# Other token pieces, sixteen places for whole weights and four stages for their splits, in an attention and two-MLP kernel

## What is computed

```python
kth = np.partition(scores, -32, axis=-1)[..., -32:-31]
scores = np.where(scores >= kth, scores, -1e9)
attn = np.exp(scores - np.max(scores, axis=-1, keepdims=True))
attn = attn / (np.sum(attn, axis=-1, keepdims=True) + 1e-09)
x = np.matmul(attn, v)                          # 2304 x 512 after the transpose
gate = 1 / (1 + np.exp(-(x @ w_gate)))          # 512 x 1536
y = (gate * (x @ w_val)) @ w_out                # 1536 x 512
r = np.maximum(y @ w_in, 0)                     # 512 x 2048
out = (r * r) @ w_out2                          # 2048 x 512
```

## Time and profile before

| | before |
|---|---|
| median of the runs shown | 1252.26 us |
| the profiled execution, own time | 1252.19 us |
| its span, first to last instruction | 1250.4 us |
| mean granted TensorE clock | 0.978 |
| PE matmul busy | 1169.2 us, 94% |
| DVE busy | 848.4 us, 68% |
| ACT busy | 740.7 us, 59% |
| POOL busy | 626.3 us, 50% |
| DMA | 270.13 MB, mean 216 GB/s |

### The profile page before, as it was taken

One profiled execution on the slowest core, in us unless ns is written; L12 is line 12 of the kernel. 1 busy time (PEld: TensorE's weight loads), 2 busy tenths in 40 slices (PEclk: granted clock), 3 DMA queues, 4 the chain that ended last, 5 costly groups with the idle time before them and its releaser, 6 DMA issues.

```text
span 1250.4 us, 21797 instructions
## 1 busy us (share of the span) xinstructions
PE 1169.2 (94%) x7520; PEld 991.9 (79%) x7520; DVE 848.4 (68%) x1756; ACT 740.7 (59%) x1758; POOL 626.3 (50%) x539
## 2 busy tenths in 40 slices
PE   3469989869999999999999999999999999999999
PEld 2248877769999898888888777777778788888999
DVE  7988988737779977788997667688864445610121
ACT  5777778557768756666776666467654443531221
POOL 4875668646648845553664445356543333530220
PEclk9769999989999999999999999999999999999999
DMA  7874667686665785655456555454555545556997
GB/s 262 313 266 143 230 209 225 204 298 225 224 228 199 246 309 192 198 199 170 160 191 230 200 168 191 168 185 153 175 193 194 178 160 181 176 189 212 365 369 263
DMA packets 89245, 270.13 MB, mean 216 GB/s; under 512 B 9904, under 2 KB 15024, under 8 KB 89136
## 3 DMA queue, kind: packets, MB, share of 16 engines
q1 hardware_dynamic: 89136, 268.74, 62.7%
HBM read 228.33 MB, written 40.37 MB: 215 GB/s over the span
## 4 chain that ended last, share of the span: by engine, by line
PE 80%; ACT 6%; POOL 4%; DMA 4%; DVE 4%; issue 2%; SPq 1%; ACTq 0%; DVEq 0%; POOLq 0%
PE ps L497 21%; PE ps L499 19%; PE ps L498 19%; PE ps L438 6%; PE ps L402 5%; PE ps L418 5%; PE ps L483 3%; DMA w_split<-ring 2%; POOL below L728 2%; DVE work L663 2%; DVE top L661 1%; POOL ring L723 1%; ACT scores L529 1%; DMA ring<-w_in 1%; ACT probs L548 1%
## 5 line engine op out<-in xcount | busy, mean ns | idle before, releaser
L728 POOL TENSOR_TENSOR below<-scores,below 128x576 f32<-128x576 f32 x144 | 205.2, 1425 | 297.9 <-ACT below L541 285.5
L661 DVE MAX8 top<-work 128x8 f32<-128x576 f32 x432 | 312.9, 752 | 5.0
L497 PE MATMUL ps<-xy_hi,ring 128*128 128x512 f32 (+3 forms) x800 | 292.1, 365 | 0.3 <-ACT act_buf L597 0.3
L499 PE MATMUL ps<-xy_hi,ring 128*128 128x512 f32 (+3 forms) x800 | 283.2, 354 | 0.0
L498 PE MATMUL ps<-xy_lo,ring 128*128 128x512 f32 (+3 forms) x800 | 283.2, 354 | 0.0
L663 DVE MATCH_REPLACE8 work<-top,work 128x576 f32<-128x576 f32 x288 | 213.8, 742 | 0.0
L497 PE MATMUL ps<-g_hi,ring 128*128 128x512 f32 (+3 forms) x560 | 203.0, 363 | 0.0
L499 PE MATMUL ps<-g_hi,ring 128*128 128x512 f32 (+3 forms) x560 | 197.8, 353 | 0.0
L498 PE MATMUL ps<-g_lo,ring 128*128 128x512 f32 (+3 forms) x560 | 197.6, 353 | 0.0
L497 PEld LDWEIGHTS ps<-xy_hi,ring 128*128 128x128 f32 x800 | 151.4, 189 | 24.8 <-issue 9.7
L687 DVE SCALAR_TENSOR_TENSOR full_buf<-act_buf,ps 128x512 f32<-128x512 f32 (+3 forms) x60 | 35.5, 591 | 193.1 <-PE ps L499 176.7
(11 more groups left out here) (56 smaller groups left out, 1749.9 us busy)
## 6 DMA issues: line engine op xcount, KB each, us to landing
ring<-w_split SPq DMA_DIRECT2D x318, 512.0 KB, 3.7
w_split<-ring SPq DMA_DIRECT2D x68, 512.0 KB, 4.2
ring<-w_in SPq DMA_DIRECT2D x113, 256.0 KB, 3.4
vt<-v_in SPq DMA_DIRECT2D x16, 480.0 KB, 5.3
heads_in<-qk_in SPq DMA_DIRECT2D x16, 336.0 KB, 4.8
vt<-v_in SPq DMA_DIRECT2D x16, 320.0 KB, 4.1
heads_in<-qk_in SPq DMA_DIRECT2D x16, 240.0 KB, 3.8
heads_in<-qk_in SPq DMA_DIRECT2D x8, 368.0 KB, 5.6
```

What stands on the lines that cost most here:

```text
L497: nc.tensor.matmul(dst, w_hi, hi[:, k, 0:WIDTH[c]], start=first, stop=False)
L499: mm = nc.tensor.matmul(dst, w_lo, hi[:, k, 0:WIDTH[c]], start=False, stop=final)
L661: nc.vector.max(out=best, in_=sc if step == 0 else wk).then_inc(sel_step[t % 2], 1)
L728: nc.gpsimd.tensor_tensor(out=below[:, t % 2, :], in0=scores[:, t % PLACES, :], in1=below[:, t % 2, :], op=ALU.subtract).then_inc(mask_don ...
```

## The change

The pieces become 128, 256, 384, 512, 512 and 512 tokens (2, 4, 6, 8, 8, 8 blocks of 64). NW = 1 names the number of pieces computed whole in float32 (it stays the first alone; x1 and the pieces of code for more of them are not used). Jobs before piece 1 (NWHOLE = 91 of them) now have 16 places of their own, of 2 KB per partition, in the same memory as the ring; their parts go to one of four stages of 4 KB, in memory of g_lo, which piece 0 does not use. The ring of 8 double places takes over from piece 1 on; job k >= 91 waits for the two whole places that its place covers. SP stores a stage three blocks after its block (STORE_LAG), ACT waits for the store of four splits before. POOL no longer waits for the block's matmuls, and waits once, in piece 1, for the last four stages' stores. probs_h has two places, and its memset is twice as long. The splits ahead of piece 0 begin in slot 0 and not in slot 2; at the start SP issues sixteen whole weights, eight before the second v and eight after it. JOBS, its number of splits (68) and of whole loads (113) stay as they are. With the pieces, MLP_AT goes from 16, 41, 69, 101, 133, 149 to 12, 29, 53, 85, 117, 149, and the groups from 32 to 36 (still 64 full and 16 half units).

```diff
-CHUNK_BLOCKS = (3, 6, 7, 8, 8, 4)
+CHUNK_BLOCKS = (2, 4, 6, 8, 8, 8)
+NW = 1
...
-RING = 8
+RING, WPLACES, STAGES = 8, 16, 4
 AHEAD = 5
+STORE_LAG = 3
+CLASSES = NW + 2
...
+NWHOLE = NPRE + NW * NB
...
+STAGED = [k for k in SPLITS if k < NWHOLE]
+STAGE_OF = {k: r for r, k in enumerate(STAGED)}
...
+RING0 = (NWHOLE + 1) % WPLACES // 2
+def ring_place(k):
+    return (k - NWHOLE + RING0) % RING
...
+def jobs_ahead(k):
+    if k < NWHOLE:
+        return [k - WPLACES] if k >= WPLACES else []
+    if k >= NWHOLE + RING:
+        return [k - RING]
+    return [i for i in range(NWHOLE - WPLACES, NWHOLE) if i % WPLACES // 2 == ring_place(k)]
+LOAD_AT = {}
+for _k in range(len(JOBS)):
+    if jobs_ahead(_k) and max(jobs_ahead(_k)) >= NPRE:
+        LOAD_AT.setdefault(max(jobs_ahead(_k)) + 1, []).append(_k)
+FIRST_LOADS = [k for k in range(NWHOLE) if not jobs_ahead(k)]
...
-    SPLIT_AT.setdefault(2 + _k // 2, []).append(_k)
+    SPLIT_AT.setdefault(min(2, MLP_AT[0] - (NPRE + 1) // 2) + _k // 2, []).append(_k)
...
-        probs_h = sb("probs_h", [P, SEQ + B64])
+        probs_h = sb("probs_h", [P, 2, SEQ + B64])
...
+        with nc.sbuf_tensor("stage", [P, STAGES, 2, KT * P], F32R) as stage, \
...
-        with nc.sbuf_tensor("ring0", [P, RING, 2, KT * P], F32) as ring0:
+        with nc.sbuf_tensor("wring", [P, WPLACES, KT * P], F32) as wring:
...
             def load_weights(k):
...
+                for ahead in jobs_ahead(k):
+                    if ahead >= NPRE:
+                        sp.wait_ge(blk_done, ahead - NPRE + 1)
+                    if JOBS[ahead][2] and ahead < NWHOLE:
+                        sp.wait_ge(w_lo_done, SPLIT_OF[ahead] + 1)
+                    elif JOBS[ahead][2]:
+                        wait_stored(sp, ahead)
...
-                    load_weights(k - 1 + RING)
-                    if k + AHEAD in SPLIT_OF and JOBS[k + AHEAD][0] == 1:
+                    for job in LOAD_AT.get(k, []):
+                        load_weights(job)
+                    if k + AHEAD in SPLIT_OF and JOBS[k + AHEAD][0] == NW:
                         store_parts(k + AHEAD)
-                    if c == 0 and k in SPLIT_OF:
-                        store_parts(k)
+                    if k - STORE_LAG in STAGE_OF and k - STORE_LAG >= NPRE:
+                        store_parts(k - STORE_LAG)
...
-            for k in range(RING):
+            for k in FIRST_LOADS[:RING]:
                 load_weights(k)
             load_v(1)
+            for k in FIRST_LOADS[RING:]:
+                load_weights(k)
...
             def split_weights(k):
-                act.wait_ge(ring_loaded[k % RING], 16 * (k // RING + 1))
-                nc.scalar.activation(place(k)[:, 0, :], whole(k), ACT.Copy).then_inc(w_hi_done, 1)
+                wait_loaded(act, k)
+                if k < NWHOLE and STAGE_OF[k] >= STAGES:
+                    wait_stored(act, STAGED[STAGE_OF[k] - STAGES])
+                nc.scalar.activation(both_parts(k)[:, 0, :], whole(k), ACT.Copy).then_inc(w_hi_done, 1)
...
                 pool.wait_ge(w_hi_done, SPLIT_OF[k] + 1)
-                if JOBS[k][0] == 0:
-                    pool.wait_ge(blk_done, k - NPRE + 1)
```

More of the change, by code:

```diff
@@ L171 @@
     HEADS_AT.setdefault(max(FIRST_TILE[_g - 1] - 3, 0), []).append(_g)
-for _c in range(1, NC):
+for _c in range(NW, NC):
     for _p in range(PAIRS):
@@ L242, in probs_of, with both_parts @@
             u, part = TILES[t]
-            return probs_h[:, 0:SEQ] if part == 2 else probs[:, RANK[u] % 2, part, :]
-        def place(k):
-            return ring[:, k % RING, :, :]
+            return probs_h[:, RANK[u] % 2, 0:SEQ] if part == 2 else probs[:, RANK[u] % 2, part, :]
         def whole(k):
-            return ring0[:, k % RING, 1, :]
+            return wring[:, k % WPLACES if k < NWHOLE else 2 * ring_place(k) + 1, :]
+        def both_parts(k):
+            return stage[:, STAGE_OF[k] % STAGES, :, :] if k < NWHOLE else ring[:, ring_place(k), :, :]
         const_step = sem("const_step")
@@ L256, in attention_mlps @@
         out_stored = [sem("out_stored0"), sem("out_stored1")]
+        whole_loaded = [sem(f"whole_loaded{i}") for i in range(WPLACES)]
         ring_loaded = [sem(f"ring_loaded{i}") for i in range(RING)]
-        w_stored = [sem(f"w_stored{i}") for i in range(RING)]
+        stage_stored = [sem(f"stage_stored{i}") for i in range(STAGES)]
+        ring_stored = [sem(f"ring_stored{i}") for i in range(RING)]
         w_hi_done = sem("w_hi_done")
@@ L293, in wait, with wait_loaded, wait_stored @@
                 eng.wait_ge(s, count)
[L295 to L301, removed]
+        def wait_loaded(eng, k):
+            if k < NWHOLE:
+                eng.wait_ge(whole_loaded[k % WPLACES], 16 * (k // WPLACES + 1))
+            else:
+                eng.wait_ge(ring_loaded[ring_place(k)], 16 * ring_use(k))
+        def wait_stored(eng, k):
+            if k < NWHOLE:
+                eng.wait_ge(stage_stored[STAGE_OF[k] % STAGES], 16 * (STAGE_OF[k] // STAGES + 1))
+            else:
+                eng.wait_ge(ring_stored[ring_place(k)], 16 * ring_stores(k))
         block = ctx.enter_context(nc.Block())
@@ L335, in store_parts @@
+                n = JOBS[k][1]
+                loaded = whole_loaded[k % WPLACES] if k < NWHOLE else ring_loaded[ring_place(k)]
+                if JOBS[k][3]:
+                    sp.dma_start(whole(k), w[n, :, :]).then_inc(loaded, 16)
+                    return
+                wait_stored(sp, STORED_BY[n])
+                sp.dma_start(both_parts(k).rearrange("p a c -> p (a c)").bitcast(F32), w_split[n, :, :]).then_inc(loaded, 16)
             def store_parts(k):
                 sp.wait_ge(w_lo_done, SPLIT_OF[k] + 1)
+                stored = stage_stored[STAGE_OF[k] % STAGES] if k < NWHOLE else ring_stored[ring_place(k)]
@@ L337, in store_parts @@
                 sp.dma_start(w_split[JOBS[k][1], :, :],
-                             place(k).rearrange("p a c -> p (a c)").bitcast(F32)).then_inc(w_stored[k % RING], 16)
+                             both_parts(k).rearrange("p a c -> p (a c)").bitcast(F32)).then_inc(stored, 16)
             def mlp_dma(blocks):
                 for c, n in blocks:
-                    kind, m, i, parts = BLOCKS[n]
+                    kind, m, i, last = BLOCKS[n][0], BLOCKS[n][1], BLOCKS[n][2], BLOCKS[n][3] - 1
@@ L351, in mlp_dma @@
+                    if kind == "out" and i == last:
                         sp.wait_ge(out_copied, c * NM + m + 1)
@@ L585, in evac @@
                 k = NPRE + c * NB + n
[L586 removed]
+                if k + AHEAD in SPLIT_OF and JOBS[k + AHEAD][0] == NW:
                     split_weights(k + AHEAD)
[L588 removed]
+                if c < NW and k in SPLIT_OF:
                     split_weights(k)
@@ L608, in evac @@
                         nc.scalar.activation(act_buf[:, t % 2, 0:n_w], acc(c, n), ACT.Copy).then_inc(out_copied, 1)
-                if c > 0 and 2 <= n <= 2 * NJ1 and n % 2 == 0:
+                if c >= NW and 2 <= n <= 2 * NJ1 and n % 2 == 0:
                     j = n // 2 - 1
@@ L612, in evac @@
                     nc.scalar.activation(g_hi[:, j, 0:n_w], full_buf[:, j % 2, 0:n_w], ACT.Copy).then_inc(gv_hi_done, 1)
-                if c > 0 and H0 < n <= OUT0:
+                if c >= NW and H0 < n <= OUT0:
                     j = n - H0 - 1
@@ L689, in evac @@
                                                    op1=ALU.mult).then_inc(gv_done, 1)
-                if c > 0 and kind == "y" and i == parts - 1:
+                if c >= NW and kind == "y" and i == parts - 1:
                     dve.wait_ge(y_hi_done, c * NM + t + 1)
@@ L720, in split_weights @@
                 pool.wait_ge(w_hi_done, SPLIT_OF[k] + 1)
-                if JOBS[k][0] == 0:
-                    pool.wait_ge(blk_done, k - NPRE + 1)
-                nc.gpsimd.tensor_tensor(out=place(k)[:, 1, :], in0=whole(k), in1=place(k)[:, 0, :].bitcast(F32),
+                nc.gpsimd.tensor_tensor(out=both_parts(k)[:, 1, :], in0=whole(k), in1=both_parts(k)[:, 0, :].bitcast(F32),
                                         op=ALU.subtract).then_inc(w_lo_done, 1)
@@ L767, in _ @@
             nc.gpsimd.memset(ident[:, :], 0.0)
-            nc.gpsimd.memset(probs_h[:, :], 0.0).then_inc(const_step, 1)
+            nc.gpsimd.memset(probs_h[:, :, :], 0.0).then_inc(const_step, 1)
             pool.wait_ge(const_step, 1)
```

114 lines of the change are left out of this document (55 added, 59 removed).

## The result

The changed kernel takes 1269.36 us (median of 4 runs, 1267.53 to 1272.06) against 1251.38 us for the kernel before beside it. The ratio is 1.0158 with a 95% interval of 1.0129 to 1.0187: 1.6% slower. The prediction had 1233 us, 1205 to 1262.

A forecast was written before the change was run, and what follows sets the result against it. DMA was taken to bound piece 0, SP's store-load loop piece 1, and PE the pieces from 2 on. 74 + 110 + 165 + 207 + 486 + 189 = 1231 us of span gave 1233 us, range 1205 to 1262.

The forecast's parts named there:

- 22.7 rounds of 7.3 us are 165: Piece 1: SP's store-and-load loop, once round per three blocks, sets the pace; 165 us against a floor of 139.
- Rival (b): Piece 1's loop stays at 9.0 us a round: 204 us, 39 more, 1272 us in all; chance 0.17.
- the loop: Piece 1: next whole load stands behind a store waiting for POOL, then ACT, then the load before; 7.3 us a round.
- Head, 74: Stretch before piece 0: slot 12 and its first matmul at 71 us, plus 3 for heads issued late behind eight more weights.
- Piece 0, 110: Piece 0, 17 slots: DMA ends it at 184 us from the start, leaving 110; floor 91 from DVE.
- the DMA's 61 MB: Loads, stores, heads and v to piece 0's end: 173 us at 352 GB/s, taken as 184 with 6% over.
- the prediction's own sign of the engines' order: Sign of being wrong: piece 0 slots over 6.5 us with DMA under 0.8 mean engines' order, not DMA.
- The floor of a narrow piece: PE's matmul needs, by distances of 0.109, 0.1198, 0.1736 and 0.2274 us, fall by only 10 us over the whole change.
- Pieces 2 to 5: Pieces set by PE: 207 us for piece 2, 486 for pieces 3 and 4, 189 for piece 5.
- The store chain: Piece 0: a block was replaced only once multiplied, split and stored; sixteen places and stages remove that wait, 28.1 us of SP.
- The Trainium skill's 425 GB/s for a lone core: DMA rate weighed against about 358; by 425 the DMA needs 144 us to piece 0's end and DVE sets it.

The follow-up runs named there:

- e1: Changed kernel with piece 1's stores of split parts issued three blocks later, behind the next whole load: 1247.1 us, ratio 0.997 to the kernel before.
- e3: Changed kernel with piece 1's stores three blocks later and the second eight weights issued behind the heads: 1242.6 us, ratio 0.994 to the kernel before.
- e2: Changed kernel with weights 9 to 16 issued two per slot in slots 0 to 3, behind the heads due there: 1261.6 us.
- e7: e4 with the splits ahead of piece 0 begun in slot 0 and not slot 2: 1236.5 us, ratio 0.987 to the kernel before.
- e10: e9 storing and loading only the high half of each split block (output not the reference's): 1237.7 us, ratio 0.988 to the kernel before.
- e9: Changed kernel with heads issued first and piece 1's store one block later: 1242.7 us, ratio 0.993 to the kernel before.
- e4: Changed kernel with the old pieces (192, 384, 448, 512, 512, 256 tokens), so the new places and stages alone: 1231.8 us, ratio 0.985 to the kernel before.
- e5: Kernel before with the new pieces, splits from slot 0 and probs_h in two places, keeping the old ring: 1311.7 us, ratio 1.048.
- e6: e4 with piece 1's store one block later, behind the whole load: 1232.1 us, ratio 0.984 to the kernel before.
- e17: e9 with two of the four matmuls of each piece 0 block left out (output not the reference's): 1247.5 us, ratio 0.997 to the kernel before.

## Why the prediction was wrong

The direction was wrong: 1233 was forecast and 1269.4 measured, 7 us beyond the range. By its own steps:

- **Piece 1, "22.7 rounds of 7.3 us are 165".** The step that failed: the mechanism was named, its price was wrong. Rival (b) with its point of decision (8.1 us a round, 184 us) was what happened: 8.52 us, 192 us. The 7.3 came from three rounds of before with a mean of 7.15. In those ACT did wait for a landing (5.36, 2.81 and 2.17 us), but they were picked from 22 intervals for being tight; the 19 quoted had 8.99, and nothing in the rows said that more than two rounds in a row could be that tight. e1 took the loop out and piece 1 fell by 22 us. Even so it took 169.5 (e1) to 172.4 us (e3), so 165 was short of what the rest of the piece asks, loop or no loop. That (b)'s 1272 us lies near 1269.4 is luck: its piece 1 was 12 us too long, and it had the head 10 too short.
- **Head, 74.** The second step that failed. Measured 84.1. The late heads were seen and priced at 3 us; they cost 7.6 (e2). DVE stood 6 us for them at tile 3, and no later slot made that good. The splits from slot 0 were not priced at all: about 5 us if e7 may be carried over, which is not shown.
- **Piece 0, 110.** Measured 113.0: near, but by luck, for the cause was wrong. The sum took the DMA's 61 MB as the bound. The head did run at 316 GB/s, but with half the split traffic piece 0 was just as long (e10). It took 113/17 = 6.6 us a slot against 5.14 for DVE alone, and PE's waits in it are for accumulators to be read. That is the prediction's own sign of the engines' order (slots over 6.5 us), only at a DMA share of 0.82 and not under 0.8. Which part of the order sets it stays open.
- **The floor of a narrow piece.** What PE must do fell by about 10 us as forecast: in the changed kernel the matmuls of an MLP start 0.112, 0.120, 0.173 and 0.227 us apart (medians at 128, 256, 384 and 512 tokens), against 0.109, 0.1198, 0.1736 and 0.2274 in the sum. But head, piece 0 and piece 1 of e9 hold 53 slots in 359 us, 6.8 a slot; those of e4 69 slots in 442, 6.4 a slot. With PE's needs of 247 and 350 us (estimates, by the prediction's distances), e9 leaves PE 112 us unused there and e4 92. The new pieces move work to where PE is the only bound and leave less beside the attention, which has its own pace.
- **Pieces 2 to 5.** 203.8, 488.8 and 188.6 us against 207, 486 and 189: right, from before's rows at the same widths.
- **The store chain.** Right: gone. The new places were worth 20 us (e4 against before) with the old pieces and 42 (e5 against the changed kernel) with the new.
- **The Trainium skill's 425 GB/s for a lone core.** The head had 316 GB/s at a share of 0.88, by estimate 359 at full share, and e9's piece 1 305 at 0.85, the same. By these rows too the lower figure of the Trainium skill ("HBM Reference", Specifications: about 358) is the nearer. But e10 shows that neither would have changed piece 0.

## What to carry to other kernels

When work is made denser, look in the slack of the present schedule for loops through a queue that works in order: a store that waits for an engine, with the next load behind it. This one cost nothing that could be measured where PE wanted 8.3 us a round (e6) and 22 us where it wanted 6.1 (e1). Its tightest rounds did not give its price, and neither does the mean of all, which holds rounds set by others. What tells is the idle time inside the loop, here ACT's in front of whole blocks (23.3 us, 4.7 without the loop), and a run with the store behind the load; that order costs nothing (e6). And of a change with two halves, measure each: here the buffers were worth 20 us and the new pieces lost 38.

## What the runs showed that was not expected

- The length of a wait says little of its price. SP waited 52 us in piece 1 for landing stores (e3) and none of it mattered (e9). 110 us of waits for POOL at the same queue went with a loss of 22 us, and 69 us of them (e9) with none that shows, the next whole load being out already.
- Leaving out half of piece 0's matmuls did not make it shorter. The granted clock of that stretch had a mean of 0.80 and not 0.98 (e17), with PE busy for 82 of 116 us; what is taken off PE came back as longer matmuls and longer waits.
- Halving the split traffic (e10) took piece 1 from 305 to 201 GB/s and gave 6 us. A DMA share of 0.85 looked like a bound and was hardly one.
